# Two joins of a three-stage kernel: where the last head pair is divided, when the sigmoid table is loaded, and when the output weights are split

## What is computed

```python
q_pool = q.reshape(B, H, S // 2, 2, D).mean(axis=3)
attn = softmax(q_pool @ k.T / sqrt(D)); x = attn @ v
h = x @ w_in;  x = (h * tanh(log1p(exp(h)))) @ w_out      # layer 0
h = x @ w_in2; y = where(h > 0, h, exp(h) - 1) @ w_out2   # layer 1
```

## Time and profile before

| | us |
|---|---|
| median of 3 runs | 681.18 (681.0 to 681.3) |
| the profiled execution, its own time | 681.34 |
| its span, first to last instruction | 679.2 |
| PE busy in that span | 653.3 |
| granted TensorE clock, mean | 1.000 |

### The profile page before, as it was taken

How to read it: one execution, slowest core, us unless ns; L and a number is a source line. 1 busy time by engine, 2 the same in 40 slices (tenths; PEclk the granted TensorE clock), 3 DMA queues, 4 the chain that set the end, 5 groups by cost and what they waited for, 6 DMA issues and landing times.

```text
span 679.2 us, 12400 instructions
## 1 busy us (share of the span) xinstructions
PE 653.3 (96%) x3984; PEld 636.6 (94%) x3984; DVE 405.3 (60%) x707; ACT 391.3 (58%) x732; POOL 420.3 (62%) x384
## 2 busy tenths in 40 slices
PE   4999999999999999989999999999999999999998
PEld 2898999998999999989999999999999999999998
DVE  7677888787787862767776666777633232223222
ACT  4688888887989887655555556554633322222221
POOL 5587787978797866587777766777544422222221
PEclk9999999999999999999999999999999999999999
DMA  6555667665657521122210001222222110001001
GB/s 182 160 167 157 181 172 196 172 175 163 182 158 206 131 71 47 59 63 62 63 32 0 0 0 46 63 63 63 64 73 66 33 46 0 0 0 47 1 1 46
DMA packets 35855, 57.91 MB, mean 85 GB/s; under 512 B 7568, under 2 KB 13024, under 8 KB 35808
## 3 DMA queue, kind: packets, MB, share of 16 engines
q1 hardware_dynamic: 35808, 57.32, 30.5%
HBM read 33.29 MB, written 2.40 MB: 53 GB/s over the span
## 4 chain that ended last, share of the span: by engine, by line
PE 68%; SPq 8%; POOL 6%; DVE 5%; issue 5%; DMA 4%; ACT 4%; POOLq 0%; ACTq 0%; DVEq 0%
PE py L566 8%; PE py L568 8%; PE py L567 8%; PE pH L551 8%; PE pH L553 8%; PE pH L552 8%; SPq L320 6%; PE ps L488 4%; PE ps L489 3%; PE po L504 3%; PE pm L474 3%; PE po L505 3%; PE po L506 3%; DMA sum_few<-o_rows 3%; DVE pl L816 2%
## 5 line engine op out<-in xcount | busy, mean ns | idle before, releaser
L1041 POOL TENSOR_TENSOR gl<-fg,gh 128x384 fp32r<-128x384 f32 x96 | 97.6, 1017 | 141.5 <-ACT gh L733 140.3
L796 DVE TENSOR_REDUCE part_max<-pm 128x1 f32<-128x384 f32 x225 | 118.1, 552 | 32.2 <-PE pm L474 28.4
L566 PE MATMUL py<-gh,wout_h 128*128 128x384 f32 x384 | 129.3, 337 | 4.5 <-POOL gl L1041 2.7
L984 POOL TENSOR_TENSOR pl<-p,ph 128x576 fp32r<-128x576 f32 x72 | 105.8, 1473 | 42.6 <-ACT p L649 42.5
L567 PE MATMUL py<-gl,wout_h 128*128 128x384 f32 x384 | 128.4, 334 | 0.0
L568 PE MATMUL py<-gh,wout_l 128*128 128x384 f32 x384 | 128.3, 334 | 0.0
L553 PE MATMUL pH<-xh,win_l 128*128 (+1 forms) x384 | 128.3, 334 | 0.0
L552 PE MATMUL pH<-xl,win_h 128*128 (+1 forms) x384 | 128.3, 334 | 0.0
L551 PE MATMUL pH<-xh,win_h 128*128 (+1 forms) x384 | 128.3, 334 | 0.0
L643 ACT ACTIVATE ph<-ps 128x576 fp32r<-128x576 f32 x144 | 93.8, 652 | 37.1 <-PE ps L489 34.8
L878 DVE RECIPROCAL fi<-fp 128x192 f32<-128x192 f32 x48 | 64.9, 1353 | 51.3 <-POOL fp L1049 51.3
(11 more groups left out here) (74 smaller groups left out, 1338.2 us busy)
## 6 DMA issues: line engine op xcount, KB each, us to landing
kh<-k_hi SPq DMA_DIRECT2D x60, 144.0 KB, 3.5
w_raw<-w_in SPq DMA_DIRECT2D x32, 256.0 KB, 2.7
w_raw<-w_out SPq DMA_DIRECT2D x32, 256.0 KB, 2.6
q_raw<-qT SPq DMA_DIRECT2D x16, 288.0 KB, 3.1
k_pack<-kP SPq DMA_DIRECT2D x16, 288.0 KB, 3.2
v_raw<-v SPq DMA_DIRECT2D x16, 288.0 KB, 4.0
kl<-k_pack SPq DMA_DIRECT2D x32, 144.0 KB, 2.4
q<-q SPq DMA_DIRECT2D x16, 144.0 KB, 2.4
```

The source lines that it names most:

```text
L566: pe.matmul(out, hi, gh[:, f % 4, :], start=(f == 0), stop=False)
L796: dve.tensor_reduce(part_max[:, par, j:j + 1], pm[:, at % 2, 0:MC], AX.X, ALU.max).then_inc(m_read, 1)
L984: pool.tensor_tensor(pl[:, ph_slot(slot, kt), :], p32[:, p32_slot(n, kt) % 3, :], ph[:, ph_slot(slot, kt), :].bitcast(F32), ALU.subtract). ...
```

## The change

In SP's program the loads of `w_out` blocks 2 and 3 of layer 0 stand ahead of `gather_inv` and `spread_inv` of the last pair. ACT gets one sigmoid of a single column ahead of the last `copy_o`. The division of the last pair moves: `invert` from behind unit 0 to behind unit 2, `finalize` from unit 2 to unit 4, ACT's `split_x` from unit 3 to unit 5, POOL's from unit 3 to unit 6, and `division_over` from unit 3 to unit 7; for this, eight units of tile 0 are written out and the loop has two rounds. In layer 1 with t = 0, ACT's `split_w`, with its wait, moves behind `exp_h`, `split_g` and `evacuate`.

```diff
@@ sync @@
             gather_sums(HEADS - 1)
             move_o(PAIRS - 1)
+            for par in range(2):
+                load_w(w_out[0][2 + par], 1, 2 + par, par)
             gather_inv(PAIRS - 1)
             spread_inv(PAIRS - 1)
...
-                with sp.Fori(1, NF // 2) as i:
+                with sp.Fori(2 if matrix == 1 else 1, NF // 2) as i:
@@ scalar @@
+            act.wait_ge(ql_done, HEADS - 1)
+            act.activation(q_sum[:, 0:1], q_sum[:, 0:1], ACT.Sigmoid)
             copy_o(HEADS - 1)
...
-                if t == 0:
-                    if layer:
-
-                        act.wait_ge(g2_done, NF * (NT - 1) + nf + 1)
-                    split_w(chunk(wout_h, nf), NF * (2 * layer + 1) + nf, f % 2)
+                if t == 0 and layer == 0:
+                    split_w(chunk(wout_h, nf), NF + nf, f % 2)
...
                     split_g(1, f, u)
                     if prior is not None:
                         evacuate(prior)
+                    if t == 0:
+
+                        act.wait_ge(g2_done, NF * (NT - 1) + nf + 1)
+                        split_w(chunk(wout_h, nf), NF * 3 + nf, f % 2)
...
-                        if base + f == 3:
-                            split_x(PAIRS - 1)
+                    if base == 0:
+                        for f in range(4):
+                            unit_step(layer, t, f, 4 + f, 1)
+                            if f == 1:
+                                split_x(PAIRS - 1)
...
-                    with act.Fori(1, 3 if end else 4) as i:
+                    with act.Fori(1 if base else 2, 3 if end else 4) as i:
@@ vector @@
-                        if base + f == 0:
+                        if base + f == 2:
                             invert(PAIRS - 1)
-                        elif base + f == 2:
-                            finalize(PAIRS - 1)
                     if base == 0:
+                        for f in range(4):
+                            unit_step(layer, t, f, 4 + f, 1)
+                            if f == 0:
+                                finalize(PAIRS - 1)
                         division_over(dve)
-                    with dve.Fori(1, 4) as i:
+                    with dve.Fori(1 if base else 2, 4) as i:
@@ gpsimd @@
-                        if base + f == 3:
-                            split_x(PAIRS - 1)
                     if base == 0:
+                        for f in range(4):
+                            unit_step(layer, t, f, 4 + f, 1)
+                            if f == 2:
+                                split_x(PAIRS - 1)
                         division_over(pool)
-                    with pool.Fori(1, 4) as i:
+                    with pool.Fori(1 if base else 2, 4) as i:
```

## The result

The changed kernel takes 683.28 us (median of 20 runs, 679.76 to 687.23), the kernel before 681.21 in the same series (median of 20, 679.41 to 682.83). The ratio is 1.0029, with a 95% interval of 1.0017 to 1.0042: slower by 2.1 us, where 0.4 us slower was forecast. The measured time lies outside the range that was given.

The account below looks back on a forecast made before the run. PE, busy 653.3 of 679.2 us, was taken as the bound, so only its waits could give time back. Terms of -1.9 and +2.3 gave +0.4 us on 681.18, so 681.6; range 679.6 to 682.8.

Parts of the forecast that it names:

- the second join: Passage from layer 0 to layer 1, around g2(48): a loss of 2.3 us, between 1.8 and 2.8.
- the slower side: Outcome class for times above 682.54 us, the median plus 0.2% (1.36 us); chance 0.23.
- Table load: End of attention, ACT: sigmoid table load moves into idle time ahead of the last `copy_o`; gain 1.28 us.
- Loop entry: Layer 0, unit 4: DVE and POOL no longer restart 0.43 us after POOL's `xl`; gain 0.43 us.
- weight blocks: Layer 0, blocks 2 and 3 loaded earlier: ACT's 1.49 us wait goes; gain 0.2 us, between 0 and 0.7.
- division: `invert`, `finalize` and `xl` at units 2, 4 and 6: zero change, between 0.8 us gain and 0.5 loss.
- Block 4: Layer 0, unit 4: ACT waits about 1.5 us for the load behind the division's DMAs, just covered; cost 0.
- Evacuation at unit 48 to 50: Layer 1, tile 2: late `split_w(2)` and `low_w(2)` delay `low_y`; g2(48) waits 3.1 us, a loss of 2.3.
- the second join was not freed: Rival: evacuation starts near 483.6, loss shrinks to 0.4 us; net -1.5, 679.7 us (678.9 with larger join gain); chance 0.17.
- the table was not loaded again: Rival: sigmoid table reloaded at layer 0's first sigmoid, 1.28 us stay; +1.7, 682.9 us; chance 0.08.
- block 4 was not late: Rival: block 4 comes 1 to 2 us later than 292.6; +1.4 to +2.4, 682.6 to 683.6 us; chance 0.13.
- the first join: Passage from attention to layer 0: gain of 1.9 us at g2(15), bounds -3.9 and +0.3.

Follow-up runs that it names:

- the order alone: Kernel before with only ACT's layer-1 order changed (weight split behind exp, gh and the evacuation): 684.84 us, ratio 1.0057 to the kernel before.
- the one with the order put back: Changed kernel with ACT's layer-1 weight split again ahead of exp, gh and the evacuation: 678.75 us, ratio 0.9955 to the kernel before.

## Why the prediction was wrong

**The step that failed** is the last sentence on the second join: "nothing gives the loss back: PE runs without waits to the end". PE did run without waits, but not at full rate. The sum priced a wait of 3.1 us by its length alone, and the half-rate stretch behind it, 1.5 to 3.2 us by the traces, was in no term, no bound and no rival. With it the sum is -2.2 + 2.1 + 1.5 to 3.2, that is +1.4 to +3.1, and the measured +2.1 (interval +1.2 to +2.9) lies in it. By the prediction's own bound, 682.54, the median of 683.28 is on the slower side. The trace of before had a granted clock of 1.00 from one end of the feed-forward stage to the other, with waits up to 1.76 us in it, and so did not show the price; a forecast of a wait longer than any in the trace should have bounded it from above by half rate for as long as it may last. The Trainium skill ("TensorE: Matmul & The Clock Gate", section "Part 1: The HAM clock gate (the "warmup" mystery)") says that the array's clock goes back to its lower level when TensorE has been idle; the traces here agree for waits of 1.84 us and more at g2(48), though not for each execution.

**Table load:** right. 1.28 forecast, 1.32 measured alone. The load fitted into the idle time ahead of `copy_o`; the one-column sigmoid took the 0.20 us assumed. The drain by which the Trainium skill ("ScalarE: Activation LUTs", section "What ACT_TABLE_LOAD costs") would have made it 2.66 does not show in the path.

**Loop entry, weight blocks, division:** the right sign, too small. 0.63 us forecast, 1.04 measured alone. The loop entry's idle 0.43 us on DVE and POOL is gone, as forecast. The 0.2 taken for the weight blocks has no support in the traces: `low_w` of block 2 fell from 1.47 to 0.68 us, but that of block 4 rose from 0.69 to 1.54, so the slow one only moved. POOL's `xl` took 1.43 in place of 1.74 us, a gain that I had in the bounds and not in the sum; but a DVE product was beside it in both kernels, and in the new place it is that product which is slow, 1.48 us. What the 1.04 us are made of is therefore open; no run takes the three parts apart. The sigmoid and these parts together give 2.22, near the sum of the two, 2.36. As forecast, the gain of unit 3 is not carried in full: g2(3) is 3.6 us earlier (22.91 against 26.48), g2(15) only 2.2.

**Block 4:** right on the wait. ACT waited 1.41 us (1.5 forecast). The cover, said to be just enough, was short by the 0.55 us that POOL stood idle ahead of `multiply_d(5)`. The kernel before had 0.62 us of the same kind ahead of `multiply_d(3)` (at 287.54), behind its wait for block 2, so this cost moved rather than came anew. What it is worth by itself was not tried.

**Evacuation at unit 48 to 50:** right. A wait of 3.1 us forecast, 3.05 measured; a loss of 2.3 forecast, 2.14 measured with the order alone and 217.14 - 214.76 = 2.38 between the changed kernel and the one with the order put back. The cause is the one named, `low_w(2)` ahead of `low_y` on DVE; putting it behind takes the loss away.

**Rivals:** the second join was not freed; the table was not loaded again; block 4 was not late. The forecast put 0.60 on the same and 0.23 on slower.

**Sums:** two are off by 0.1 us, and nothing hangs on them. The lower bound of the first join, 2.70 + 1.1, is -3.8 and not -3.9; and the steps from the evacuation to g2(48) add up to 3.54, not 3.45, which makes that loss 2.5 in place of 2.3.

## What to carry to other kernels

Before work is moved later in one engine's order, look at the order of the engine that reads it: here ACT's late weight split was waited for by a DVE instruction that stood ahead of the one PE needed, and putting these two DVE steps the other way round was worth the whole loss. Where a change may make PE wait longer than any wait in the same stage of the old trace, price the wait and a stretch at half rate behind it: here 1.5 to 3.2 us beside a wait of about 3. Work that is moved to a later unit of a stage bound by that same chain is largely charged again where it lands, and so is a wait: here the wait for a block and the slow `low_w` both came back two units later. The clear gain was what left the chain, the table load.

## What the runs showed that was not expected

TensorE's granted clock fell to 0.5 around g2(48) with PE waits of 1.84, 2.73, 3.03 and 3.05 us, for 3.4 us, and with waits of 3.02 us for 6.8. It did not fall behind waits of 0.44 to 0.95 us, nor behind 1.74 to 1.78 us at g2(3). What separates 1.78 us at one place from 1.84 at another is not settled. The changed kernel's fastest execution, 679.76 us, is the only one of the twenty with a mean clock of 1.000.

A mean clock over the span does not find this drop, since the kernel's start weighs in it differently from trace to trace. In nine of the thirteen traces the view has a half-rate stretch of 6.8 us or more at 14 to 26 us; in the other four, the kernel before among them, it has 1.00 there. But the products of the kernel before, 0.24 us apart at 24.4 us and 0.13 us apart at 29.1, show that PE ran at about half pace there too. So a 1.00 in the first 27 us of these traces is not to be relied on, and neither is a difference of 0.005 or so between two mean clocks. The stages view over 4 us around g2(48) does show the drop.

```profile
24.38 0.44 PE L488 MATMUL ps<-q,kh 128*128 128x288 f32 x1
24.62 0.44 PE L489 MATMUL ps<-q,kl 128*128 128x288 f32 x1
...
29.06 0.29 PE L489 MATMUL ps<-q,kl 128*128 128x288 f32 x1
29.19 0.29 PE L488 MATMUL ps<-q,kh 128*128 128x288 f32 x1
```
